# Attention and two expert layers on one core: the last two accumulation steps are split, and a branch that the run skips gets shorter

## The reference

```python
h = x @ w_in                                   # 512 -> 2048
g = np.where(pos, h, np.where(neg, 0.0, (h + beta) ** 2 / (4.0 * beta)))
y = g @ w_out                                  # 2048 -> 512
```

## Time and profile before

| | |
|---|---|
| median of 3 runs | 545.35 us (545.23 to 545.76) |
| profiled execution, its own time | 546.15 us |
| its span, first to last instruction | 541.5 us |
| mean granted TensorE clock | 0.973 of full speed |
| PE, DVE, POOL, ACT busy | 520.1, 250.2, 211.6, 206.2 us |

### The profile page before, as it was taken

How to read it: one execution, slowest core, us unless ns; L and a number is a source line. 1 busy time by engine, 2 the same in 40 slices (tenths; PEclk the granted TensorE clock), 3 DMA queues, 4 the chain that set the end, 5 groups by cost and what they waited for, 6 DMA issues and landing times.

```text
span 541.5 us, 9204 instructions
## 1 busy us (share of the span) xinstructions
PE 520.1 (96%) x3555; PEld 450.0 (83%) x3556; DVE 250.2 (46%) x585; ACT 206.2 (38%) x451; POOL 211.6 (39%) x242
## 2 busy tenths in 40 slices
PE   6889999999999999999999999999999999999993
PEld 3677888889998888888888888888899988898892
DVE  6956566533226435646535547452322573222221
ACT  4953655642322324443423443432332223322221
POOL 1656788762222324544533535552222333221220
PEclk9777999999999999999999999999999999999998
DMA  8991201003001104201210420000300081740003
GB/s 249 348 383 63 68 30 47 30 2 116 1 1 50 63 24 161 73 4 36 86 44 18 145 75 30 4 0 21 116 1 1 0 312 43 254 153 1 2 0 119
DMA packets 19298, 42.95 MB, mean 79 GB/s; under 512 B 2116, under 2 KB 3856, under 8 KB 19252
## 3 DMA queue, kind: packets, MB, share of 16 engines
q1 hardware_dynamic: 19124, 42.32, 22.9%
q0 software_dynamic: 128, 0.02, 0.0%
HBM read 33.01 MB, written 9.57 MB: 79 GB/s over the span
## 4 chain that ended last, share of the span: by engine, by line
PE 89%; DVE 6%; issue 1%; POOL 1%; DMA 1%; ACT 1%; SPq 0%; DVEq 0%; ACTq 0%; POOLq 0%
PE bank L957 37%; PE bank L973 34%; PE bank L832 4%; PE bank L796 4%; PE bank L813 3%; PE bank L850 2%; PE bank L842 1%; DVE row_sum L1116 1%; DVE bank L1099 1%; PE bank L986 1%; DVE row_max L1104 1%; PE bank L906 1%; DMA qk<-in_qk_dram 1%; PE bank L887 1%; DVE prob_first L1090 1%
## 5 line engine op out<-in xcount | busy, mean ns | idle before, releaser
L1685 POOL TENSOR_TENSOR g_lo<-act_f,g_hi 128x384 fp32r<-128x384 f32 x96 | 97.1, 1012 | 204.8 <-ACT g_hi L1571 204.4
L1562 ACT ACTIVATE act_f<-act_f,half_col 128x384 f32<-128x384 f32 x96 | 59.2, 617 | 209.3 <-DVE act_f L1314 209.1
L1314 DVE TENSOR_SCALAR act_f<-bank 128x384 f32<-128x384 f32 x96 | 53.3, 556 | 163.1 <-PE bank L957 160.9
L957 PE MATMUL bank<-x_hi,win_hi 128*128 128x384 f32 x384 | 91.7, 358 | 0.0
L1571 ACT CAST g_hi<-act_f 128x384 fp32r<-128x384 f32 x96 | 49.2, 512 | 94.6 <-DVE act_f L1317 94.2
L957 PE MATMUL bank<-x_hi,win_lo 128*128 128x384 f32 x384 | 85.1, 341 | 0.0
L973 PE MATMUL bank<-wout_hi,g_hi 128*128 128x512 f32 x282 | 84.9, 410 | 0.0
L957 PE MATMUL bank<-x_lo,win_hi 128*128 128x384 f32 x384 | 84.4, 339 | 0.0
L973 PE MATMUL bank<-wout_hi,g_lo 128*128 128x512 f32 x282 | 80.3, 393 | 0.0
L973 PE MATMUL bank<-wout_lo,g_hi 128*128 128x512 f32 x282 | 80.2, 393 | 0.0
L1317 DVE TENSOR_TENSOR act_f<-act_f,bank 128x384 f32<-128x384 f32 x96 | 52.3, 545 | 40.0 <-ACT act_f L1562 38.3
(11 more groups left out here) (131 smaller groups left out, 481.7 us busy)
## 6 DMA issues: line engine op xcount, KB each, us to landing
w_early<-in_w_dram SPq DMA_DIRECT2D x4, 2048.0 KB, 9.1
qk<-in_qk_dram SPq DMA_DIRECT2D x12, 592.0 KB, 4.0
out_dram<-y_rows SPq DMA_DIRECT2D x18, 256.0 KB, 2.6
y_dram<-y_rows SPq DMA_DIRECT2D x18, 256.0 KB, 2.8
win_raw<-in_w_in_dram SPq DMA_DIRECT2D x16, 256.0 KB, 9.7
wout_raw<-in_w_out_dram SPq DMA_DIRECT2D x16, 256.0 KB, 9.8
v<-in_v_dram SPq DMA_DIRECT2D x6, 384.0 KB
v<-in_v_dram SPq DMA_DIRECT2D x6, 288.0 KB
```

Source lines behind the costliest of these rows:

```text
L957: mm = pe.matmul(h_ps[s % 2][:, 0:CH], w[:, f, P * k:P * (k + 1)], x[:, k, cols], start=(at == 0), stop=(at == len(order) - 1))
L1314: dve.tensor_scalar(tile, h_ps[s % 2][:, 0:CH], -1.0, 1.0, ALU.max, ALU.min).then_inc(clip_ready, 1)
L1562: act.activation(tile, tile, ACT.Square, bias=half_col[:, 0:1], scale=0.5).then_inc(square_ready, 1)
L1685: pool.tensor_tensor(g_lo[:, s % RING, :], act_f[:, s % 2, :], g_hi[:, s % RING, :].bitcast(F32), ALU.subtract).then_inc(g_lo_ready, 1)
```

## The change

Three edits.

1. `last_outputs`: step 94 goes through the usual `output(94)`, product by product over the three tiles, behind its own semaphores. Only step 95 goes tile by tile, and only step 95 waits for g_hi and g_lo of step 95.
2. `for_tiles`: the two copies of the body ahead of the loop are gone. The loop starts at 0 instead of 2, and its even and odd bodies are the only ones.
3. `store_rows` no longer stores the last chunk's rows into `y_dram`. `first()` inside the branch does it, with a semaphore of its own, `y_kept`. The counts that wait for `y_stored` are lowered by 16.

```diff
-                body(0, 0, n_tiles)
-                with eng.If(n_tiles > 1):
-                    body(0, 1, n_tiles)
-                with eng.If(n_tiles > 2):
-                    with eng.Fori(2, SLOTS_UP, SPAN) as span:
-                        with eng.If(span < n_tiles):
-                            with eng.Fori(0, SPAN, 2) as i:
-                                with eng.If(span + i < n_tiles):
-                                    body(span + i, 0, n_tiles)
-                                    with eng.If(span + i + 1 < n_tiles):
-                                        body(span + i, 1, n_tiles)
+                with eng.Fori(0, TILES_UP, SPAN) as span:
+                    with eng.If(span < n_tiles):
+                        with eng.Fori(0, SPAN, 2) as i:
+                            with eng.If(span + i < n_tiles):
+                                body(span + i, 0, n_tiles)
+                                with eng.If(span + i + 1 < n_tiles):
+                                    body(span + i, 1, n_tiles)
...
                     sp.dma_start(out[rows, :], y_rows[:, t, :]).then_inc(y_stored[t], 16)
-                    sp.dma_start(y_dram[rows, :], y_rows[:, t, :]).then_inc(y_stored[t], 16)
+                    if c < CHUNKS - 1:
+                        sp.dma_start(y_dram[rows, :], y_rows[:, t, :]).then_inc(y_stored[t], 16)
...
             def first():
+                for t in range(CT):
+                    rows = slice(CH * (CHUNKS - 1) + P * t, CH * (CHUNKS - 1) + P * (t + 1))
+                    sp.dma_start(y_dram[rows, :], y_rows[:, t, :]).then_inc(y_kept, 16)
...
             for t in range(CT):
-                sp.wait_ge(y_stored[t], 32 * CHUNKS)
+                sp.wait_ge(y_stored[t], 32 * (CHUNKS - 1) + 16)
...
-                for s in range(STEPS - LAG, STEPS):
-                    pe.wait_ge(g_hi_ready, s + 1)
-                    pe.wait_ge(g_lo_ready, s + 1)
+                for s in range(STEPS - LAG, STEPS - 1):
+                    output(s)
+                s, f = STEPS - 1, FT - 1
+                pe.wait_ge(g_hi_ready, STEPS)
+                pe.wait_ge(g_lo_ready, STEPS)
                 for t in range(CT):
-                    for s in range(STEPS - LAG, STEPS):
-                        f = s % FT
-                        for i, (w, g) in enumerate([(wout_hi, g_hi), (wout_lo, g_hi), (wout_hi, g_lo)]):
-                            mm = pe.matmul(y_ps[t][:, :], g[:, s % RING, P * t:P * (t + 1)], w[:, f, :],
-                                           start=False, stop=(f == FT - 1 and i == 2))
+                    for i, (w, g) in enumerate([(wout_hi, g_hi), (wout_lo, g_hi), (wout_hi, g_lo)]):
+                        mm = pe.matmul(y_ps[t][:, :], g[:, s % RING, P * t:P * (t + 1)], w[:, f, :],
+                                       start=False, stop=(i == 2))
                     if t < CT - 1:
                         mm.then_inc(rows_done, 1)
-                mm.then_inc(l2_done, LAG)
+                mm.then_inc(l2_done, 1)
```

More of the change, by code:

```diff
@@ L35 @@
 SLOTS_UP = 2 + -(-(SLOTS - 2) // SPAN) * SPAN
+TILES_UP = -(-SLOTS // SPAN) * SPAN
 FAR = float(1 << 17)
@@ L401, in build @@
         tile_expert = sb("tile_expert", [1, SLOTS_UP], F32)
-        tile_expert_i = sb("tile_expert_i", [1, SLOTS_UP + SPAN], I32)
+        tile_expert_i = sb("tile_expert_i", [1, TILES_UP + SPAN], I32)
         n_tiles_i = sb("n_tiles_i", [1, 1], I32)
@@ L456, in build @@
         y_act, y_dve = sem("y_act"), sem("y_dve")
+        y_kept = sem("y_kept")
         y_stored = [sem(f"y_stored{t}") for t in range(CT)]
@@ L1716, in first @@
                 for t in range(CT):
-                    pool.wait_ge(y_stored[t], 32 * CHUNKS)
+                    pool.wait_ge(y_stored[t], 32 * (CHUNKS - 1) + 16)
+                pool.wait_ge(y_kept, 16 * CT)
                 for i in range(2):
```

## The result

The changed kernel takes 540.31 us (median of 4 runs, 539.54 to 541.67), the kernel before 545.56 us (4 runs, 545.23 to 546.23). The ratio is 0.9917, 95% interval 0.9898 to 0.9936: 0.8% faster, 4.5 us, about twice the 2.1 us of the forecast and outside its range.

The account below looks back on a forecast made before the run. PE was taken to bound the kernel, its end being products, flags, `left_i`, register load, jump and drain. Gains of 1.60 + 0.5 + 0 = 2.1 us took the median from 545.35 to 543.25 us, range 542.3 to 544.2.

Parts of the forecast that it names:

- The split: Last products on PE: step 94 no longer waits for step 95, so all that follows comes 1.60 us earlier.
- The stores and the jump: PE's jump at the end: fewer stores let its instruction packet come sooner, worth 0.5 us (between 0 and 0.8).
- The length of the branch: Skipped code on PE, 1,027 instructions before and 608 after: priced at 0, the jump still waits.
- rival (a): PE's jump at the end becomes free, some 0.07 us, and SP is last: 540.75 us, chance 0.08.
- The 4.6 us outside the span: Time outside the profiled execution's span: claimed to stay at 4.6 us, with no gain from it.
- Rival (b): End of PE's code: the target falls across a packet's edge, PE waits for a second packet: 547.3 us, chance 0.04.

Follow-up runs that it names:

- e1: The kernel before with only the split of the last products (step 94 as usual, step 95 tile by tile): 544.39 us, ratio 0.9994.
- e8: The kernel before with the split and the moved stores, still four copies of the body in the branch: 543.41 us, ratio 0.9970.
- e2: The kernel before with only the shorter branch (two copies of the body instead of four): 542.25 us, ratio 0.9962.
- e5: The kernel before with 47 dead matmuls (94 instructions) added on PE inside the branch that is not entered: 542.02 us, ratio 0.9941.
- e6: The changed kernel with PE's tile body in the branch cut to one semaphore, so PE jumps over 185 instructions instead of 608: 538.03 us.
- e4: The changed kernel with 82 dead matmuls (164 instructions) added on PE inside the branch that is not entered: 543.11 us, ratio 0.9969.
- e12: The changed kernel with 78 dead matmuls (156 instructions) added on PE inside the branch that is not entered: 540.83 us, ratio 0.9934.
- e11: The changed kernel itself, unaltered, measured and profiled again: 541.46 us, ratio 0.9930 to the kernel before.
- e7: The changed kernel with a prefetch hint on PE, ahead of the last products, for the comparing branch over the general loop: 540.66 us.
- e9: The changed kernel with PE's condition turned round and the prefetch hint given to the now unconditional branch: 539.94 us, ratio 0.9916.
- e10: The changed kernel with PE's general loop in the middle, jumped over ahead of step 94's products, the last products behind it: 537.83 us.

## Why the prediction was wrong

The direction was right, the size was half of it.

**The split: right.** 1.60 us forecast, 1.68 measured. Step 94's products began 0.53 us ahead of the mark, as worked out, and DVE's 0.74 us for each tile was the new limit. The small rest comes from L988's matmuls: eight of them took 0.228 us each ((530.47 - 528.65) / 8), not 0.234.

**The stores and the jump: right in kind, and a coupling missed.** I took 0.5 us, and the profiled pair shows 0.70. With the stores out of the way the packet begins 1.0 us after the jump; in the kernel before it was 1.6, at 538.76, which is 0.6 behind the stretch that I had it follow at once. What the forecast didn't see is that the split alone would run its products into the same stores. Terms that are added must be free of each other, and these two weren't (e1, e8). How well 0.5 was sized can't be said: with the same six stores the jump took 4.03, 3.47 (e2) and 3.81 us (e5), which makes the gain of 3.33 anything from 0.14 to 0.70.

**The length of the branch: right about the jump, wrong about the price.** The jump still waits; by the count PE's target lies outside its block and the next, and e6 shows that a target inside costs 0.37 us. I had rival (a) at 540.75 us, and the measured 540.31 is close to it, but its mechanism didn't occur: the jump took 3.33 us, not 0.07. A matching total is no evidence for a mechanism.

**The step that failed** is this one: "The 4.6 us outside the span of the profiled execution (546.15) and the 0.8 us by which it is above the median are not touched." With it failed the price of 0 for edit 2. What lies outside the span fell from 4.4 us in the mean to 2.1, and edit 2 alone does that (e2). By these runs, the code behind the branch of the kernel before ends so close to a block's edge that what runs at the end crosses it and waits for a fetch; edit 2 moved it away. That the place counts and not the length is shown in both directions: e5 took the loss away with more code, e4 and e12 brought one back, and e8, without edit 2, kept it. For the kernel before itself the packet is in the trace, but no instruction behind the span is, so which one waits for it is argued, while the 2.3 us themselves are measured. Rival (b) was the right mechanism with the sides exchanged: I feared the edge for the changed kernel, and it was the kernel before that had it. My own count put its target 62 instructions from the next edge, and I gave that no price. I had counted the instructions and could place them only within thirty, yet the case that before was the one paying had no chance of its own.

**The sum** for the profiled pair: 1.68 + 0.70 in the tail and 4.6 - 2.1 outside is 4.9 us. The ratio says 4.5, with e11 3.8. The difference lies within the 2 us by which spans of one kernel differ. Inside the span the forecast's 2.1 us were about right: 2.4 by the tails, and 1.4 by the mean spans of e11 and of before on its chip (538.98 and 540.36).

## What to carry to other kernels

Look at the sequencers' rows behind the last computed value, and at the gap between time and span: here PE's jump and that gap were 8.6 of the last 10.2 us, and the chain of waits named neither. Code that is never executed has a price by where it puts the code behind it. Jump over it where the engine still has queued work, and before an idle-time gain is added to a transfer's, try both together, since one may run into the other.

## What was not expected of the hardware

- By the count of instructions, a jump to the block that follows PE's own took 0.37 us (e6), one beyond it 3.3 to 3.5 us in the seven kernels whose packet came 1.0 us after the jump (the changed one, e4, e7, e8, e9, e10, e12), and up to 4.79 us behind stores (e1).
- PE's sequencer was far enough ahead of its array that a jump of 3.3 us left no hole in the products (e10).
- Running over a block's edge soon after such a jump cost 3.2 us in the barrier (e4), and with the edge 8 instructions further on 0.9 us in the mean, outside the span (e12).
- A prefetch hint ahead of the last eighteen products changed the jump by less than 0.1 us, at both kinds of branch, and no instruction packet followed it (e7, e9).
